# Double buffers for the upper probabilities, two regrouping buffers for three, and value sums one slot earlier

## The reference

```python
# q (2, 12288, 128), kv (2, 384, 32, 128), w_sr (128, 128)
kv_pool = kv.reshape(B, H // 4, 4, W // 4, 4, C).mean(axis=(2, 4))
k = v = kv_pool.reshape(B, -1, C) @ w_sr          # 768 keys per batch
s = (q @ k.transpose(0, 2, 1)) / sqrt(C)
a = exp(s - s.max(-1)); a /= a.sum(-1) + 1e-09
x = (a @ v).reshape(-1, C)
h = x @ w_in;  x = (h * cos(h)) @ w_out            # first network
h = x @ w2_in; out = (h * sigmoid(1.702 * h)) @ w2_out
```

## Time and profile before

| what | value |
|---|---|
| median of 3 runs | 2679.44 us (2677.34 to 2682.35) |
| the profiled execution's own time | 2679.44 us |
| its span | 2677.7 us |
| PE, DVE, ACT, POOL busy | 97%, 78%, 70%, 81% of the span |
| mean granted TensorE clock | 0.992 of full |
| chain that ended last | PE 80%, SPq 10%, DMA 5%, DVE, issue, POOL and ACT 1% each |
| DMA share by slice (40 slices of 67 us) | 7988888850101101..., so 0.7 to 0.9 in the first eight |

### The profile page before, as it was taken

The page is one execution under the profiler, slowest core; times in us unless marked ns, Lnnn a source line. Parts: engine busy times, 40 slices in busy tenths (PEclk is TensorE's granted clock), DMA queues, the critical chain, the costliest instruction groups (busy, mean ns, idle before and its releaser), DMA issues.

```text
span 2677.7 us, 37678 instructions
## 1 busy us (share of the span) xinstructions
PE 2594.7 (97%) x11797; PEld 2139.9 (80%) x11797; DVE 2076.1 (78%) x2264; ACT 1876.6 (70%) x2280; POOL 2172.9 (81%) x1830
## 2 busy tenths in 40 slices
PE   8998888889999999999999999999999999999999
PEld 6777766767888888888888888888888888888887
DVE  7777777777787777777777878787877787877876
ACT  4655666667777777777777777777777777777776
POOL 2776888879888888888888888888888888888873
PEclk9999999989999999999999999999999999999999
DMA  7988888850101101000101010100101000100000
GB/s 245 296 283 283 260 265 267 276 178 9 24 12 23 23 12 24 12 24 12 24 12 24 12 24 12 24 23 12 24 12 24 12 24 12 24 12 24 12 16 12
DMA packets 191147, 193.88 MB, mean 72 GB/s; under 512 B 113457, under 2 KB 138353, under 8 KB 190065
## 3 DMA queue, kind: packets, MB, share of 16 engines
q1 hardware_dynamic: 190032, 193.03, 24.6%
q10 hardware_dynamic: 1056, 0.13, 0.0%
HBM read 92.34 MB, written 63.01 MB: 58 GB/s over the span
## 4 chain that ended last, share of the span: by engine, by line
PE 80%; SPq 10%; DMA 5%; DVE 1%; issue 1%; POOL 1%; ACT 1%; POOLq 0%
PE psum L691 26%; PE psum L692 26%; PE psum L693 26%; SPq L475 7%; DMA gathered<-bounce 3%; SPq L469 1%; POOL g_lo L676 1%; DMA bounce<-turned 1%; DMA bounce<-turned_last 1%; PE psum L763 1%; DVE neg_max L1259 1%; PE psum L765 1%; ACT probs_t_hi L1057 1%; DVE turned L1271 0%; SPq L479 0%
## 5 line engine op out<-in xcount | busy, mean ns | idle before, releaser
L676 POOL TENSOR_TENSOR g_lo<-g,g_hi 128x512 fp32r<-128x512 f32 x768 | 1120.0, 1459 | 67.7 <-ACT g_hi L1174 7.6
L1392 DVE TENSOR_TENSOR g_lo<-g,g_hi 128x1024 fp32r<-128x1024 f32 (+1 forms) x396 | 643.4, 1625 | 433.3 <-ACT g L1169 432.0
L1167 ACT ACTIVATE g_hi<-psum 128x1024 fp32r<-128x1024 f32 (+1 forms) x396 | 397.3, 1003 | 558.8 <-PE psum L693 558.7
L673 POOL CAST g_hi<-g 128x512 fp32r<-128x512 f32 x750 | 565.1, 753 | 229.8 <-DVE g L1383 229.8
L691 PE MATMUL psum<-x_hi,w_lo 128*128 128x512 f32 x1536 | 598.6, 390 | 1.3 <-DVE g L1383 1.3
L691 PE MATMUL psum<-g_hi,w_lo 128*128 128x512 f32 x1536 | 597.9, 389 | 0.8 <-POOL g_lo L676 0.8
L692 PE MATMUL psum<-x_lo,w_hi 128*128 128x512 f32 x1536 | 598.1, 389 | 0.0
L693 PE MATMUL psum<-x_hi,w_hi 128*128 128x512 f32 x1536 | 598.0, 389 | 0.0
L692 PE MATMUL psum<-g_lo,w_hi 128*128 128x512 f32 x1536 | 597.5, 389 | 0.0
L693 PE MATMUL psum<-g_hi,w_hi 128*128 128x512 f32 x1536 | 597.5, 389 | 0.0
L1383 DVE TENSOR_TENSOR g<-psum,g 128x512 f32<-128x512 f32 x768 | 490.0, 677 | 1.9 <-ACT g L1160 1.8
(11 more groups left out here) (87 smaller groups left out, 2493.0 us busy)
## 6 DMA issues: line engine op xcount, KB each, us to landing
gathered<-bounce SPq DMA_DIRECT2D x48, 768.0 KB, 5.4
bounce<-turned SPq DMA_DIRECT2D x64, 384.0 KB, 6.2
gathered<-turned SPq DMA_DIRECT2D x256, 96.0 KB, 2.8
bounce<-turned_last SPq DMA_DIRECT2D x32, 384.0 KB, 6.2
gathered<-turned_last SPq DMA_DIRECT2D x128, 96.0 KB, 3.1
x_dram<-x_out SPq DMA_DIRECT2D x48, 256.0 KB, 5.1
x_raw<-x_dram SPq DMA_DIRECT2D x48, 256.0 KB, 2.6
x_inv<-inverse_dram SPq DMA_DIRECT2D x48, 256.0 KB, 3.4
```

The costliest lines, as they stand in the source:

```text
L673: nc.gpsimd.tensor_copy(g1_hi[at][:, t], g1[at][:, t]).then_inc(g1_hi_ready, 1)
L676: nc.gpsimd.tensor_tensor(g1_lo[at][:, t], g1[at][:, t], g1_hi[at][:, t].bitcast(F32), ALU.subtract).then_inc(g1_lo_ready, 1)
L1167: nc.scalar.activation(g2_hi[ring2(j, p)][:, t], h2[buffer2(j)][:, t], ACT.Silu, scale=GELU)
L1392: nc.vector.tensor_tensor(g2_lo[ring2(j, p)][:, t], g2[ring2(j, p)][:, t], g2_hi[ring2(j, p)][:, t].bitcast(F32), ALU.subtract).then_inc(g ...
```

## The change

It does four things at once. The upper part `probs_t_hi` gets two buffers, taken in turn by chunk. The `turned` buffers go from three to two (`turned_last` is gone, and its place in memory is taken by the second `probs_t_hi`), so that the first turn of chunk c now waits for the regrouping of chunk c-2. The waits for `upper_summed` and `lower_made` ahead of a rounding are replaced by one wait for the value sums of chunk c-2. And the value sums on TensorE start one slot earlier, at 4c+9; the slots of the roundings stay at 4c+8 and 4c+9.

```diff
-    HI_SLOT, LO_SLOT, VALUES_SLOT, STORE_SLOT = 8, 9, 10, 15
+    HI_SLOT, VALUES_SLOT, STORE_SLOT = 8, 9, 15
...
-    probs_t_hi = put("probs_t_hi", [P, KT, TOK], F32R)
+    probs_t_hi = [put(f"probs_t_hi{n}", [P, KT, TOK], F32R) for n in range(2)]
-    turned_last = put("turned_last", [P, KT * TOK], F32)
...
             def regroup(c):
-                b, n = c // CB, c % 3
+                b, n = c // CB, c % 2
...
-                dst, src = gathered[b][n], turned[b][n]
+                dst, src = gathered[b][c % 3], turned[b][n]
...
-                sp.wait_ge(bounced[n], BOUNCED * (c // 3 + 1))
+                sp.wait_ge(bounced[n], BOUNCED * (c // 2 + 1))
...
             def round_probabilities(c):            # GpSimd
-                pool.wait_ge(regrouped[c % 3], REGROUPED * (c // 3 + 1))
-                if c >= 1:
-                    pool.wait_ge(upper_summed, (c - 1) * PARTS + BY_POOL + 1)
-                    lower_made(pool, c - 1, BY_POOL)
+                pool.wait_ge(regrouped[c % 2], REGROUPED * (c // 2 + 1))
+                if c >= 2:
+                    pool.wait_ge(values_summed, c - 1)
...
-            for s in range(LO_SLOT, TILES):
-                c, i = divmod(s - LO_SLOT, SUB)
+            for s in range(VALUES_SLOT, TILES):
+                c, i = divmod(s - VALUES_SLOT, SUB)
...
             def sum_upper(c, i):                   # TensorE
-                last.then_inc(upper_summed, 1)
...
-            for i in (PARTS - 1, PARTS):
-                sum_values(CHUNKS - 3, i)
+            sum_values(CHUNKS - 3, PARTS)
...
             def round_probabilities(c, i):         # ScalarE
                 if i == 0:
-                    act.wait_ge(regrouped[c % 3], REGROUPED * (c // 3 + 1))
-                if c >= 1:
-                    act.wait_ge(upper_summed, (c - 1) * PARTS + i + 1)
-                    lower_made(act, c - 1, i)
+                    act.wait_ge(regrouped[c % 2], REGROUPED * (c // 2 + 1))
+                    if c >= 2:
+                        act.wait_ge(values_summed, c - 1)
...
             def turn(s):                           # VectorE
-                if j == 0 and c >= 3:
-                    dve.wait_ge(regrouped[c % 3], REGROUPED * (c // 3))
-                dst = turned[c // CB][c % 3][:, :, :, j * BLK:(j + 1) * BLK]
+                if j == 0 and c >= 2:
+                    dve.wait_ge(regrouped[c % 2], REGROUPED * (c // 2))
+                dst = turned[c // CB][c % 2][:, :, :, j * BLK:(j + 1) * BLK]
```

More of the change, by code:

```diff
@@ L174, in attention_and_networks @@
                                  turned_at[b] + n * CHUNK_BYTES))
-        turned[b].append(turned_last[:, :].rearrange("p (f k t) -> p f k t", f=GROUPS, k=KT))
         for n in range(3):
@@ L323, in attention_and_networks @@
     turned_made = sem("turned_made")
-    bounced = [sem(f"bounced{n}") for n in range(3)]
-    regrouped = [sem(f"regrouped{n}") for n in range(3)]
-    upper_summed = sem("upper_summed")
+    bounced = [sem(f"bounced{n}") for n in range(2)]
+    regrouped = [sem(f"regrouped{n}") for n in range(2)]
     probs_hi_ready = sem("probs_hi_ready")
@@ L375, in upper_part @@
     def upper_part(c, i):
-        return probs_t_hi[:, part_tiles(i), :].rearrange("p k (a t) -> p a k t", a=GROUPS)
+        return probs_t_hi[c % 2][:, part_tiles(i), :].rearrange("p k (a t) -> p a k t", a=GROUPS)
     def by_tile(x, order):
@@ L391, in upper_made @@
                            c * BY_POOL + i + 1 + (PARTS - BY_POOL if c == CHUNKS - 1 else 0))
[L393 to L398, removed]
     def split_of(i):
@@ L762, in sum_upper @@
                 for t in range(KT)[part_tiles(i)]:
-                    nc.tensor.matmul(x1_ps[c % 2], v_lo[b][:, t, :], probs_t_hi[:, t, :],
+                    nc.tensor.matmul(x1_ps[c % 2], v_lo[b][:, t, :], probs_t_hi[c % 2][:, t, :],
                                      start=t == 0, stop=False)
-                    last = nc.tensor.matmul(x1_ps[c % 2], v_hi[b][:, t, :], probs_t_hi[:, t, :],
-                                            start=False, stop=False)
-                last.then_inc(upper_summed, 1)
+                    nc.tensor.matmul(x1_ps[c % 2], v_hi[b][:, t, :], probs_t_hi[c % 2][:, t, :],
+                                     start=False, stop=False)
             def sum_lower(c, part):
@@ L773, in sum_lower @@
                     if t % PART_TILES == 0:
-                        lower_made(pe, c, t // PART_TILES)
+                        i = t // PART_TILES
+                        if (c, i) in LAST_LO:
+                            pe.wait_ge(last_lo_ready, LAST_LO.index((c, i)) + 1)
+                        else:
+                            pe.wait_ge(probs_lo_ready, c * PARTS + i + 1)
                     last = nc.tensor.matmul(x1_ps[c % 2], v_hi[b][:, t, :],
```

## The result

The changed kernel takes 2704.88 us (median of 4 runs, 2704.63 to 2710.16) against 2680.59 us before: ratio 1.0097, 95% interval 1.0080 to 1.0114, so slower: by 24.3 us as the medians differ, by 26 us as the ratio has it. The forecast was 2694, range 2681 to 2716. The profiled execution took 2708.19 us, 3.3 above the median, with a span of 2706.4, 28.7 more than that of before.

The account below looks back on a forecast made before the run. SyncE's gapless queue was taken to bound the attention, TensorE the networks. Terms +10 (chunks 13 to 43), +1 (first stage), +3 (last chunks), +1 (clock and DMA relief) made +15 on 2679.4: 2694 us, range 2681 to 2716.

Parts of the forecast that it names:

- The third turned buffer is in use: On VectorE, chunk 25's first turn ran at 302.91 us with two regroupings open; with two buffers it would move to 309.00.
- X: Way from a gather's landing through the held turns to SyncE's next regrouping but one: 8.6 us, against 7.3 before.
- SyncE's line 469 waits for VectorE in most chunks: Sign expected in SyncE's queue in the profile after: waits for VectorE of some 0.5 us each.
- A: SyncE's regrouping of a chunk, from its start to the issue of the gather: 8.97 us.
- landing 5.5: Time from the gather's issue on SyncE to the use of its data: 5.5 us in the loop over two chunks.
- +10 us from chunk 13 to 43: Attention's middle: loop of 11.55 us per chunk against a mean of 11.31, +7 us, plus about 3 for partly absorbed stalls.
- The clock: TensorE behind the rounding's wait: slow spells in one chunk in six more, +5 us, against -4 from relieved DMA engines: +1.
- The rival in which every chunk starts cold: TensorE's upper sums at half clock in every chunk, 0.75 us per chunk, +32 us: 2721 us; chance 0.09.
- The last chunks: Chunk 47 would reach SyncE at 565.6 us instead of 562.60, delaying the networks' start: +3 us.
- The start: First stage, to about 130 us, held by the DMA engines at 0.94 busy: +1 us at most.
- the hidden case: Rival: the turns' 4.4 us to spare hide the wait and SyncE's queue stays the bound: 2682 us, 2678 to 2685; chance 0.20.
- Two upper buffers at nothing: Second upper buffer and removed waits ahead of the rounding: cost and gain 0, since the gather was the last wait.

Follow-up runs that it names:

- two_turned: The kernel before with two turned buffers for three and nothing else of the change: 2689.47 us, ratio 1.0029.
- Round_first: The changed kernel with ScalarE's first rounding of a chunk put ahead of the exponential of its slot: 2703.22 us, ratio 1.0088.
- before_offload: The kernel before with the store of a chunk's result and the load of queries issued by ScalarE instead of SyncE: 2661.04 us, ratio 0.9917.

## Why the prediction was right, point by point

*SyncE's queue bounds the attention before.* Shown: taking 0.9 us of issues a chunk from it gives 20 us.

*The third turned buffer is in use; the first turn would wait for the landing.* Right: 33 of 39 first turns start with the landing. VectorE idles for it 30 times, 1.6 us in the mean, for the 2 to 4 us of the forecast.

*X would be 8.6 us.* Measured 9.64 (8.91 from GpSimd's rounding). The way to the end of the last turn was right (8.50 us worked out, 8.13 in the rows above, 8.59 the median from the first turn's start). Without the earlier sums I had 7.2, which was too small as well: two_turned has 8.52. The last link was wrong: I took SyncE to start behind the turn. It starts behind the load of queries, which needs the transposes, and these stand behind the second upper sums since the sums moved by one slot. I had counted the queue's issues but not what each of them waits for. So the sign of "SyncE's line 469 waits for VectorE in most chunks" failed too: that wait is at line 445. Round_first shortens only the turns' way, and by the turns alone it would have taken the loss away; it didn't, until the queries moved too. In six chunks VectorE itself comes 1.0 to 3.2 us late to the held turn, which the forecast did not have either.

*A 8.97 and landing 5.5.* The regrouping up to the gather fell to 8.46 (median of before 8.80), the gather landed in 5.2 (5.4 in the earlier trace rows). The relief of the DMA engines was larger than the 0.1 us I allowed. With X the three make two periods by their definition: 9.64 + 8.46 + 5.2 = 23.3 us or 11.65 per chunk (the median period of chunks 13 to 43 is 11.62). That this is near the 23.1 us forecast is partly luck: X was 1.0 us too small and the other two terms together 0.8 us too large.

*+10 us from chunk 13 to 43.* This is the term that was mis-sized: 24.1 us. I set a typical loop of 11.55 against a mean of 11.31 that held the stalls of the weight loads, and gave 3 us for what the loop would not absorb. Like with like it is 11.55 against 10.94, +18 us over 30 chunks; the measured medians, 11.62 and 10.94, make it 20.4. The stalls at chunks 18 and 32 are there in full in both (15.3 and 13.4 us before, 15.4 and 14.2 after). The 24.1 us are also of an execution that is 3.3 us above the median of its kernel.

*The clock.* Six more periods than before are over 13 us (chunks 20, 22, 23, 26, 33 and 37). Five of the six start right behind a spell at 1.2 GHz, and 23 is the next after 22. The rest between 20.4 and 24.1 lies in such long periods, and shorter ones behind them give part back. The rival in which every chunk starts cold did not come: the granted clock is 0.96 for 0.97. Whether a spell is the cause or only the company of a late landing stays open.

*The last chunks*: +3 forecast, +2.0 measured. *The start*, where I had only +1: +2.8 to chunk 3 and +1.3 to chunk 13; chunk 2 came 14.32 us behind chunk 1, where it came 11.1 before, with a spell at 50.5 us.

*The range.* 2704.88 lies inside it, 11 us above the forecast, partly by luck: the upper end of 2716 came from a regrouping of 9.7 and a landing of 6.0 us, and both got shorter instead of longer. What took the time up was the mis-sized +10 above. The lower end, 2681, is one less than the sum of the hidden case, 2682.

*Two upper buffers at nothing*: right as far as it could be tried. *Sums one slot earlier*: right, nothing by themselves (1.0008) and part of the loss in the chain. But I put the two turned buffers without them at no loss, and they cost 0.29%. TensorE then waits for the queries' split behind the held turn, 60.4 us, and that may be where it goes; no run takes this wait away alone, so the cause of the 0.29% stays open.

## What to carry to other kernels

When a buffer is taken away, find the loop that its wait closes and add up the in-order neighbours of the waiting instruction: the wait for the landing itself cost 0.1%, at most 0.2%, once its neighbours were moved, and what stood behind it on ScalarE and TensorE cost the rest. Follow each issue of a queue without gaps to what it waits for, not only its length; a small load of queries that the change doesn't touch became the last wait. And compare a typical period with a typical one, not with a mean that holds stalls.

## What the runs showed of the hardware

A copy of 96 KB issued by SyncE takes 0.6 us (median of line 475) and up to 2.5 us (at 435.47 us in the trace of before); moving other issues away made the regrouping longer, 9.24 us for 8.80, at a DMA share of 0.91 for 0.88. ScalarE issues transfers beside its work at about the same price: the queries' load took 0.37 us in before_offload, for 0.42 us on SyncE in the kernel before (medians). TensorE's clock fell to 1.2 GHz behind an idle 1.88 us in the trace of before and did not behind 2.68 us; the first of these is

```profile
343.66 0.72 PE L763 MATMUL psum<-probs_t_hi,v_lo 128*128 128x512 f32 x1 [1.88 <-ACT probs_t_hi L1057]
344.19 0.63 PE L765 MATMUL psum<-probs_t_hi,v_hi 128*128 128x512 f32 x1
```
